# Linear attention and two expert layers on one core: TensorE's groups of a chunk in another order

## What is computed

```python
state = np.zeros((B, H, D, D), dtype=np.float32)
for t in range(S):
    state = gamma[None, :, None, None] * state + np.einsum('bhd,bhe->bhde', k[:, :, t], v[:, :, t])
    y[:, :, t] = scale * np.einsum('bhd,bhde->bhe', q[:, :, t], state)
...
logits = x @ w_gate
e_idx = np.argmax(logits, axis=1)
```

## Time and profile before

| | us |
|---|---|
| median of 3 runs | 604.64 |
| lowest, highest | 604.48, 605.7 |
| profiled execution | 605.38 |
| its span in the trace | 603.70 |
| attention part, 4 to 126 us: TensorE busy | 115.58 of 122 |
| TensorE busy, whole span | 547.0 |

### The profile page before, as it was taken

How to read it: one execution, slowest core, us unless ns; L and a number is a source line. 1 busy time by engine, 2 the same in 40 slices (tenths; PEclk the granted TensorE clock), 3 DMA queues, 4 the chain that set the end, 5 groups by cost and what they waited for, 6 DMA issues and landing times.

```text
span 603.7 us, 10700 instructions
## 1 busy us (share of the span) xinstructions
PE 547.0 (91%) x4349; PEld 443.6 (73%) x4349; DVE 251.6 (42%) x422; ACT 197.1 (33%) x372; POOL 135.7 (22%) x145
## 2 busy tenths in 40 slices
PE   4999999944999999999999999999999999756893
PEld 3777777723899889889889889889889889611441
DVE  2456666465124444353363363254263351211343
ACT  2224242211123444344354253354264261301032
POOL 2314142204311141151141042042040031020000
PEclk9999999985799999999999999999999999969696
DMA  8899888512136327418318305405403407779949
GB/s 314 287 345 375 313 323 296 197 52 81 42 113 228 141 82 261 141 49 295 141 33 309 141 8 195 141 4 200 140 6 141 139 5 293 284 280 377 387 149 350
DMA packets 45265, 115.61 MB, mean 191 GB/s; under 512 B 4821, under 2 KB 5358, under 8 KB 45230
## 3 DMA queue, kind: packets, MB, share of 16 engines
q1 hardware_dynamic: 36654, 99.83, 46.0%
q0 software_dynamic: 4688, 8.21, 4.4%
q10 hardware_dynamic: 3888, 7.08, 3.1%
HBM read 101.26 MB, written 13.84 MB: 191 GB/s over the span
## 4 chain that ended last, share of the span: by engine, by line
PE 76%; issue 7%; DMA 6%; DVE 5%; POOL 2%; SPq 2%; ACT 1%; DVEq 0%; POOLq 0%; ACTq 0%
PE bank L1238 18%; PE bank L1239 17%; PE bank L1240 17%; PE ybank L1215 3%; PE bank L1422 3%; DMA v_units<-in_v 2%; PE bank L1183 2%; POOL k_decayed L515 2%; PE ybank L1309 2%; DMA out<-orow 1%; PE bank L1158 1%; PE ybank L1333 1%; PE bank L1251 1%; DMA xg<-x_rows,token_of_row 1%; PE bank L1196 1%
## 5 line engine op out<-in xcount | busy, mean ns | idle before, releaser
L1238 PE MATMUL bank<-xT_hi,w_hi 128*128 128x448 f32 x256 | 99.0, 387 | 1.1 <-DVE xT_lo L918 1.1
L1238 PE MATMUL bank<-hT_hi,w_hi 128*128 128x448 f32 x256 | 95.5, 373 | 0.0
L1239 PE MATMUL bank<-xT_lo,w_hi 128*128 128x448 f32 x256 | 94.8, 370 | 0.0
L1240 PE MATMUL bank<-xT_hi,w_lo 128*128 128x448 f32 x256 | 94.3, 368 | 0.0
L1240 PE MATMUL bank<-hT_hi,w_lo 128*128 128x448 f32 x256 | 93.7, 366 | 0.0
L1239 PE MATMUL bank<-hT_lo,w_hi 128*128 128x448 f32 x256 | 93.5, 365 | 0.0
L923 DVE SCALAR_TENSOR_TENSOR hT_lo<-bank,hT_hi 128x448 fp32r<-128x448 f32 x64 | 40.0, 625 | 122.0 <-ACT hT_hi L658 122.0
L538 POOL DMA_INDIRECT slot_logits<-lcur,logit_row_of_row x32 | 30.4, 949 | 205.3 <-DVE lcur L932 150.8
L658 ACT ACTIVATE hT_hi<-bank 128x448 fp32r<-128x448 f32 x64 | 34.9, 545 | 107.5 <-PE bank L1240 106.8
L1238 PEld LDWEIGHTS bank<-xT_hi,w_hi 128*128 128x128 f32 x256 | 48.9, 191 | 11.7 <-issue 6.5
L662 ACT ACTIVATE yT<-bank 128x448 f32<-128x448 f32 x32 | 17.5, 545 | 111.5 <-PE bank L1240 111.5
(11 more groups left out here) (176 smaller groups left out, 694.3 us busy)
## 6 DMA issues: line engine op xcount, KB each, us to landing
w_raw<-in_w SPq DMA_DIRECT2D x64, 512.0 KB, 6.4
v_units<-in_v SPq DMA_DIRECT2D x13, 2048.0 KB, 15.1
qk<-in_qk SPq DMA_DIRECT2D x24, 512.0 KB, 4.1
kv<-in_kv SPq DMA_DIRECT2D x24, 512.0 KB, 5.4
x_rows<-xrow ACTq DMA_DIRECT2D x27, 256.0 KB, 2.9
out<-orow SPq DMA_DIRECT2D x12, 512.0 KB, 4.4
v<-in_v SPq DMA_DIRECT2D x2, 2048.0 KB, 18.5
v_units<-in_v SPq DMA_DIRECT2D x2, 1024.0 KB, 15.7
```

The costliest lines, as they stand in the source:

```text
L1238: pe.matmul(out, wh, xh, start=first_, stop=False)
L1239: pe.matmul(out, wh, xl, start=False, stop=False)
L1240: return pe.matmul(out, wl, xh, start=False, stop=last_)
```

## The change

TensorE's groups of a chunk stand in another order: scores; q times state; gates and transposes; gate sum; k times v; the whole masked product. The waits for xT (s_y) and for the state (s_S) stand ahead of the last pair of scores in every chunk but a batch's first. s_kvd is raised by the last matmul of k times v. No matmul is added or removed, and VectorE, ScalarE, GpSimd and SyncE keep their instructions and their order.

```diff
-                        if c == CH - 1 and a_ == PAIRS - 1:
+                        if c > 0 and a_ == PAIRS - 1:
                             pe.wait_ge(s_y, i + 1)
                             pe.wait_ge(s_S, bt * (CH - 1) + c + 1)
...
+                    if c > 0:
+                        for a_ in range(PAIRS):
+                            for n in range(2):
+                                h_ = slice(n * HD, (n + 1) * HD)
+                                pe.matmul(y_at(a_, n), state[h_, a_, :], qk[par][h_, 0, a_, :],
+                                          start=(a_ < 2), stop=False, skip_group_check=True)
+                    gates(i)
+                    gate_sum(i)
+                    pe.wait_ge(s_kv[par], 16 * n_par)
                     if c < CH - 1:
-                        pe.wait_ge(s_kv[par], 16 * n_par)
-                        if c > 0:
-                            pe.wait_ge(s_y, i + 1)
-                            pe.wait_ge(s_S, bt * (CH - 1) + c + 1)
                         pe.wait_ge(s_kd, bt * (CH - 1) + c + 1)
...
-                    if c > 0:
...
-                    if c < CH - 1:
                         mm.then_inc(s_kvd, 1)
-                    else:
-                        pe.wait_ge(s_kv[par], 16 * n_par)
-                    gates(i)
                     for n in range(2):
-                        if n == 1:
-                            gate_sum(i)
                         pe.wait_ge(s_m, 2 * i + n + 1)
```

## The result

The changed kernel takes 613.21 us (median of 4 runs, 612.49 to 614.12) against 605.02 for the kernel before (4 runs, 604.48 to 605.7): ratio 1.0136, 95% interval 1.0117 to 1.0154. The forecast was 609.3 with a range of 605.9 to 613.5. The direction holds, the size is 8.2 us where 4.7 were added up. All four executions of the changed kernel lie above the 612 up to which the prediction let its own case (A) reach, and within 1.1 us of the upper end of its range.

A forecast was written before the change was run, and what follows sets the result against it. TensorE's own stream was taken to set the pace, 4.84 us a regular chunk. Terms -1.3 - 0.6 - 1.05 + 2.7 + 2.65 + 0.8 + 1.5 gave +4.7 on 604.64: 609.3 us, range 605.9 to 613.5.

The forecast's parts named there:

- case (A): The forecast itself: 609.3 us, between 606.5 and 612 with the bounds of load pauses, first chunk and clock falls; chance 0.48.
- seams: Pauses of TensorE's weight loads, 0.17 to 0.20 us at most changes of matmul group; fewer expected in the new order.
- The term for the clock: TensorE idle while VectorE splits weights in attention: one fall of the granted clock taken, +1.5 us.
- rival C: In attention, the clock falls at three or four of the waits behind weight splits: 613.8 us on; chance 0.15.
- The pair that no row showed: K-v product straight before the masked product: no load pause expected, 0.55 us instead of 0.62 from start to start.
- Rival D: Load pauses stay where same-shape groups meet, because semaphore waits make them: regular chunk 5.12, total 615.5 us; chance 0.07.
- The wait in the scores: Waiting for xT before the last scores, in all chunks but a batch's first: 1.36 us for 1.09.
- The moved state: State add at 4.05 us delays splits and xT in batches 2 and 3: fourth chunks +2.7, sixth +2.65 in all.
- no GpSimd work beside them: Fifth chunk's weight splits in batches 2 and 3 run without GpSimd work alongside and take 2.35 us.
- The first chunk: First chunk of all: k-v product moves from the shadow of wg's load to behind the gates, +0.8 us.

## Why the forecast was right, and where it was too small

The mechanism of the waits and of the seams was right. The term for the clock was not: the prediction named as a sign of being wrong that the clock falls more than once or twice, and it fell three times, which is its rival C (chance 0.15). That the number lies within the range, 0.3 below its end, is partly luck: C had priced three falls too high, at 613.8 on, and regular chunks gained more than forecast.

- **Seams.** Right: they go where shapes stay the same. The pair that no row showed, the k-v product and the masked product, was mis-sized: taken at 0.55 from start to start, measured 0.46, because the masked loads start before the last k-v loads end. That is why regular chunks gained 0.14 instead of 0.09. Rival D is out: the same semaphore waits stand ahead of these groups, and 0.46 and 4.69 leave no room for seams there. The rule of the Trainium skill cited with it (TensorE: Matmul & The Clock Gate, Part 3: Packing small matmuls) does not describe these records: both products use the full 128 rows, and the loads of the masked product start 0.46 behind the first matmul of k times v, whose matmuls are recorded as busy for 0.69 (their ends are modelled).
- **The wait in the scores.** Right, 0.27; shown by itself by the run with only the wait moved.
- **The moved state.** Right: the add came 4.03 into the chunk (forecast 4.05), the splits at 4.37 (4.39), and three of the four waits ended 3.17, 2.75 and 3.18 into their chunks (forecast 3.15, 2.73, 3.15). The chunks follow: 6.92 for 6.96, and 6.04 with the idle time filled for 5.99. The 4.05 owes a little to luck: k times v took 0.46 to the next group and not the 0.62 of the sum, and the add came 0.36 behind that group's start and not 0.24.
- **GpSimd beside the second pair of splits.** A part that was mis-sized. I wrote "no GpSimd work beside them". In batch 3 the next batch's k_decayed started 0.45 after the splits, and the pair took 3.20 instead of 2.35: TensorE waited 2.66, not 1.8. Before, GpSimd's k_decayed started only when they were over (93.01; the splits ran from 90.69 for 2.35). It starts when kv lands, so it is a matter of where the transfers stand. 0.85 us, once.
- **The clock.** The term that failed in size: one fall at 1.5 was taken, three happened. Each cost 1.4 to 1.5 us: 8.34 against 6.92 in the fourth chunks, 7.52 against 6.04 and 8.32 against 6.89 in the sixth. That is 4.3 us in place of 1.5, and 2.8 is what the sum missed of the 7.55; GpSimd's 0.85 and the larger gain of the other chunks cancel. The price of one was right. Rival C named three falls and put them at 2.0 each, too much. The reading that nothing in attention idles so long also leaves out the first chunk, where loads pause for 4.37 us and are slow behind it.
- **The first chunk.** +0.70 for +0.8. The gates started at 11.21, when wg was there, and the k-v product ran behind them with slow loads (0.94, as in the earlier trace rows). The number is partly luck: with the same instructions, the start of fast loads moved from 14.79 to 19.60 between two profiled executions, and the second chunk of batch 1 took 6.65 for 4.84.
- Together: -1.89 - 0.54 - 1.24 + 2.64 (fourth chunks) + 3.59 (sixth, with the 0.85) + 0.70 + 4.3 = +7.6, which is the distance at the gates of the last output. The median came out 3.9 above the forecast: 2.9 by the chunks, less 0.4 behind attention, 1.1 because the profiled executions lie on opposite sides of their medians, and 0.4 because the kernel before was at 605.02 in the runs compared, not at 604.64.

That the falls come from idle time is shown by the run with filled waits. Why three of four waits led to a fall and not the first (2.23 long, as the third) stays open. In the kernel with the wait behind all scores, waits of 1.94 led to a fall twice, and those of 1.51, 1.74 and 2.36 did not. So length alone does not decide it.

## What to carry to other kernels

A matmul group that moves takes its semaphore with it: ask what the released engine does next, and what is queued behind that. Here a gain of 0.14 us in each chunk was outweighed by four places where a late state pushed optional work ahead of the one result that TensorE needs; behind that result the same work costs nothing. Put groups with the same operand shape next to each other, and price an idle time of TensorE of about 2 us with the clock it may cost: of nine waits of 1.5 to 2.7 us in two kernels five led to a fall, and the three in the changed kernel cost 1.4 to 1.5 us each. My estimate for one such wait is thus five ninths of that, 0.8 us.

## What was new about the chip

- Loads of a group run under the last matmuls of the group before when both have the same shape (128 rows by 64 columns): 0.46 from start to start for 16 loads that take 0.55. Where the shape changes, the loads pause: 0.17 to 0.20 at the boundaries that show a bracket, 0.07 (k times v to q times state) to 0.12 (gate sum to k times v or masked product) at others.
- The granted clock fell to 0.50 for stretches of 3.3 us and a little more although TensorE was busy in all of them, behind waits of 1.81, 1.94 (twice), 2.23 and 2.66 us. Behind waits of 1.51, 1.74, 2.23 and 2.36 it stayed, as it did behind all of 1.32 or less.
- VectorE's pair of splits takes 2.35 us alone, 2.77 beside GpSimd's two operations (the second, k_decayed, then takes 2.02 instead of 1.05), and 3.20 beside a k_decayed that starts 0.45 into it and takes 1.67. In the kernel with the wait behind all scores one k_decayed started 1.44 into a pair: the pair kept its 2.35, and k_decayed took 1.81.
- How long TensorE's loads stay slow at the start differs between executions of the same instructions: the first group of fast loads starts at 14.79 us in one and at 19.60 in another, while the granted clock reads 1.00 in both.
